# Two GpSimd drains in the expert blocks, and the second routing's constants made in the setup: one core of Trainium2

## The chip, the cores and the metric

The kernel runs on one core of a Trainium2 chip. The metric is device time in microseconds (us), taken over whole executions. The engines that matter here are TensorE (PE in the profile, its weight loads PEld), VectorE (DVE), ScalarE (ACT), GpSimd (POOL) and SyncE (SP), which issues most DMAs. A name with a q (POOLq) is an engine's sequencer: waits, branches and drains are handled there.

## The reference

Attention over 4 batches, 8 heads, 768 positions and head size 64, banded with 8 global and 96 local keys; its output is read as 3072 tokens of width 512. Two mixture-of-experts layers follow, each with 8 experts of 512x1024 and 1024x512:

```python
# layer 1: only tokens with x @ w_skip > 0, each to its argmax expert
h = np.maximum(xc[mask] @ w1[e], 0.0)
y[mask] = gate_w[mask, None] * (h @ w2[e])     # out = x + y
# layer 2: greedy over all (token, expert) logits in falling order,
# each expert takes cap = N // E = 384 tokens
order = np.argsort(-flat)
for idx in order: ...                          # assigned[tok] = e
out[mask] = np.maximum(x[mask] @ w1[e], 0.0) @ w2[e]
```

## The kernel before

The program is three blocks, one after the other. At the end of a block every engine executes a drain (it holds until the engine's older work is done) and then meets the others in a barrier; the next block starts behind it.

**Attention (block opened under L344, ends at L192).** GpSimd does nothing here but make constants, 32 small instructions, each chained to the next by a semaphore. They end with lane_grid (L405). Then it reads a flag, branches and drains.

**First experts (ends at L741).** VectorE routes the tokens, then 8 blocks of 256 rows follow, one for each expert, and behind them smaller overflow blocks of 128 rows where an expert has more than 256 tokens. The inputs here have one overflow block. All row traffic is indirect DMA issued by GpSimd in a fixed order of code: gather(k) fetches the rows of block k, scatter(k) writes its outputs (x_rows in the profile), z_scatter(k) writes the second layer's gate logits (gate_logits). The end of GpSimd's code reads: gather(E), z_scatter(E - 2), scatter(E - 1), z_scatter(E - 1), then for the overflow block scatter(E) and z_scatter(E), then waits until all have landed.

**Second experts (ends at L1371).** SyncE loads the logits back (L1478). VectorE reduces them to their largest and smallest value (L1907 to L1909), then bests() picks each token's best open expert (L1779 to L1784), needs() and three tries search a threshold with counts on TensorE, and the first expert, its token list (listed) and its weights follow from it. The 8 stretches k = 0 to 7 then run: GpSimd gathers the rows of k (L1521), issues four accumulating DMAs that make the low parts of w2 (L1533, w2_low_part), gathers for k + 1, and scatters outputs (L1527) tile by tile. During stretch k the search for expert k + 1 goes on beside the products.

**The constants of the second routing.** GpSimd makes them at the start of this block, L1498 to L1513, 17 instructions in a chain on the semaphore filled. VectorE waits for all 17 before its first bests(), TensorE before its first count. Among them are onesb and firstb, of which the program already holds equal tiles (onesb1, firstb1) from the setup.

Of the kernel before, what the change touches and what calls it, by code (L numbers as in the profile page):

```python
# [20 lines left out]
BF16 = mybir.dt.bfloat16  # L21
I32 = mybir.dt.int32
U32 = mybir.dt.uint32
AX = mybir.AxisListType
# [93 lines left out]
def build(nc, qT, kT, kI, vL, vG, n_global, n_local, w_gate1, w1a, w2a, w_gate2, w1b, w2b, flips, steps, out, x_dram, x1_dram, z_dram):  # L118
    with ExitStack() as ctx:
# [28 lines left out]
        rows2 = sb("rows2", [P, E, CAP // P], I32)  # L148
        late = ExitStack()
# [42 lines left out]
        with ExitStack() as st:  # L192
# [173 lines left out]
            def _(pool):  # L366
# [38 lines left out]
                keep_link(g.iota(lane_grid[:], [[1, P], [0, NT]], base=0, channel_multiplier=0, **iota))  # L405

# [334 lines left out]
        with ExitStack() as st:  # L741
# [128 lines left out]
            def _(pool):  # L870
# [55 lines left out]
                z_scatter(E - 2, 0)  # L926
                scatter(E - 1, 1)
# [443 lines left out]
        with ExitStack() as st:  # L1371
# [20 lines left out]
            firstb = tb("firstb", [P, E], BF16)  # L1392
            best, bestm, cmp1, pen, owner, rank1, high = (tb(x, [P, NT]) for x in ("best", "bestm", "cmp1", "pen", "owner", "rank1", "high"))
# [4 lines left out]
            left, shut, need, cnt, alive, value = (tb(x, [P, E]) for x in ("left", "shut", "need", "cnt", "alive", "value"))  # L1398
# [3 lines left out]
            fullf = tb("fullf", [P, CANDS], BF16)  # L1402
            onesb, after = tb("onesb", [P, P], BF16), tb("after", [P, P], BF16)
            lane1 = tb("lane1", [P, P], BF16)
            steps_f = tb("steps_f", [P, TRIES, CANDS])
            ids, idsf = tb("ids", [P, NT, 2], BF16), tb("idsf", [P, 2, NT])
# [19 lines left out]
            z_loaded, ended, turned, spread, filled = (sem(x) for x in ("z_loaded", "ended", "turned", "spread", "filled"))  # L1426
# [14 lines left out]
            PHASES, FILLS = E - 1, 17  # L1441
# [52 lines left out]
            def _(pool):  # L1494
                g = nc.gpsimd
                link = Chain(pool, filled)
                iota = dict(allow_small_or_imprecise_dtypes=True)
                link(g.memset(onesb[:], 1.0))  # L1498
                link(g.memset(fullf[:], 0.0))
                link(g.memset(pen[:], 0.0))  # L1500
                link(g.memset(owner[:], 0.0))
                link(g.memset(left[:], float(CAP)))
                link(g.memset(shut[:], 0.0))
                link(g.tensor_copy(firstb[:], first[:]))
                link(g.tensor_copy(alive[:], first[:]))
                for r in range(TRIES):
                    link(g.tensor_scalar(steps_f[:, r, :], lane[:, 0:CANDS], float(CANDS) ** -(r + 1), None, ALU.mult))
                link(g.tensor_tensor(masked[:, 0:P // E, :].rearrange("p t e -> p (t e)"), before[:], ident[:], ALU.add))
                link(g.tensor_scalar(after[:], masked[:, 0:P // E, :].rearrange("p t e -> p (t e)"), -1.0, None, ALU.add))
                link(g.tensor_scalar(lane1[:], lane[:], 1.0, None, ALU.add))  # L1510
                link(g.iota(idsf[:, 0, :], [[P, NT]], base=0, channel_multiplier=0, **iota))
                link(g.iota(idsf[:, 1, :], [[0, NT]], base=0, channel_multiplier=1, **iota))
                link(g.tensor_copy(ids[:], idsf[:].rearrange("p c t -> p t c")))  # L1513
                assert link.n == FILLS
# [21 lines left out]
                for k in WINDOWS:  # L1536
                    if k:
                        scatter(k - 1, TT - 1)
                    for i in range(FC // 2):
                        w2_low_part(k, i)  # L1540
                    if k < E - 1:
                        gather(k + 1)
                    for t in range(TT - 1):
                        scatter(k, t)
# [15 lines left out]
            def _(pe):  # L1560
# [93 lines left out]
                pe.wait_ge(filled, FILLS)  # L1654
# [117 lines left out]
            def _(dve):  # L1772
# [4 lines left out]
                def bests():  # L1777
# [335 lines left out]
```

## Time and profile before

| | us |
|---|---|
| median of 3 timed executions | 887.18 |
| lowest, highest of them | 886.32, 887.83 |
| the profiled execution, its own time | 885.47 |
| span of the profiled execution (first to last instruction) | 883.7 |
| mean granted TensorE clock | 0.944 of full speed |
| PE busy | 760.9 (86%) |
| DVE busy | 537.1 (61%) |
| ACT busy | 457.4 (52%) |
| POOL busy | 166.0 (19%) |

The profiled execution's own time stands 1.8 us over its span, since launch and end lie outside the span, and 1.7 us under the median. Busy shares are averages over three blocks; a block's ends are read from its timeline. Drains are no busy time in the profile: they stand only in the list of one line's instructions.

### The profile page before, as it was taken

What the parts mean: (1) busy time and instruction counts of PE and PEld (TensorE: products, weight loads), DVE (VectorE), ACT (ScalarE), POOL (GpSimd) and SP (SyncE); (2) the same over time, 40 slices, a digit from 0 to 9 for tenths busy, and PEclk for the clock granted to TensorE, in tenths of its full rate; (3) what the DMA queues carried; (4) which work ended last, traced back from release to release, by engine and by line L of the source; (5) the groups of instructions that cost most, each with busy time, mean ns of one, the idle gap of its engine ahead of it and who ended that gap; (6) DMA issues with size and microseconds to landing.
All of it is one profiled execution on the core that took longest, in us unless ns stands there. A gap on an engine that the chain in (4) does not pass through costs nothing. (4 is left out here: it accounts for less than half of the span.)

```text
span 883.7 us, 15444 instructions
## 1 busy us (share of the span) xinstructions
PE 760.9 (86%) x5529; PEld 693.0 (78%) x5529; DVE 537.1 (61%) x1441; ACT 457.4 (52%) x919; POOL 166.0 (19%) x186
## 2 busy tenths in 40 slices
PE   0899999999559999999999514999998989999994
PEld 0799999999559898999999413888887878789793
DVE  3977777776566875667655157665665757574310
ACT  2789888988424553445544003535454443536350
POOL 5000000000021121212221111131414231322321
PEclk9999999999869999999999655999999999999998
DMA  8888999997465445645443006667575766769651
GB/s 180 176 199 216 255 211 277 216 274 207 148 226 194 146 147 195 217 171 175 159 166 115 5 5 226 149 208 171 187 192 182 188 191 174 195 176 295 186 108 39
DMA packets 66041, 157.93 MB, mean 179 GB/s; under 512 B 11158, under 2 KB 14614, under 8 KB 65952
## 3 DMA queue, kind: packets, MB, share of 16 engines
q1 hardware_dynamic: 54240, 121.05, 46.8%
q0 software_dynamic: 11712, 35.73, 16.7%
q8 instruction: 51, 0.84, 0.4%
q14 instruction: 38, 0.31, 0.1%
HBM read 119.11 MB, written 23.50 MB: 161 GB/s over the span
## 5 line engine op out<-in xcount | busy, mean ns | idle before, releaser
L1606 PE MATMUL r_ph<-r_xh,r_w1h 128*128 128x384 f32 x256 | 92.0, 360 | 0.0
L557 ACT ACTIVATE pr<-pr,nmx 128x232 f32<-128x232 f32 (+1 forms) x192 | 79.9, 467 | 17.2 <-DVE nmx L653 17.2
L1606 PE MATMUL r_ph<-r_xh,r_w1l 128*128 128x384 f32 x256 | 87.7, 343 | 0.0
L1606 PE MATMUL r_ph<-r_xl,r_w1h 128*128 128x384 f32 x256 | 87.4, 342 | 0.0
L992 PE MATMUL m_ph<-m_xh,m_w1h 128*128 128x256 f32 (+1 forms) x288 | 85.1, 295 | 0.8 <-DVE m_hl L1194 0.7
L1117 ACT ACTIVATE m_hh<-m_ph 128x256 fp32r<-128x256 f32 (+1 forms) x72 | 26.8, 372 | 111.2 <-PE m_ph L992 111.2
L992 PE MATMUL m_ph<-m_xl,m_w1h 128*128 128x256 f32 (+1 forms) x288 | 82.9, 288 | 0.0
L992 PE MATMUL m_ph<-m_xh,m_w1l 128*128 128x256 f32 (+1 forms) x288 | 82.8, 287 | 0.0
L430 PE MATMUL sc<-kk,qh 128*128 128x256 f32 x192 | 58.8, 328 | 23.8 <-DVE ql L631 23.8
L653 DVE CUSTOM_DVE_ANT_0 pr<-sc,bias 128x232 f32<-128x232 f32 (+1 forms) x192 | 64.9, 374 | 19.2 <-PE sc L431 18.7
L1620 PE MATMUL r_py<-r_w2h,r_hh 128*128 128x512 f32 x192 | 76.4, 398 | 0.0
L564 ACT ACTIVATE prt<-tp 128x384 f32<-128x384 f32 (+1 forms) x128 | 65.2, 535 | 20.4 <-PE tp L443 17.0
L1620 PE MATMUL r_py<-r_w2h,r_hl 128*128 128x512 f32 x192 | 74.9, 390 | 0.0
L1620 PE MATMUL r_py<-r_w2l,r_hh 128*128 128x512 f32 x192 | 74.8, 390 | 0.0
L1903 DVE SCALAR_TENSOR_TENSOR r_hl<-r_ph,r_hh 128x384 fp32r<-128x384 f32 x64 | 35.3, 556 | 61.9 <-ACT r_hh L1723 61.2
L471 PE MATMUL op<-vo,prt 128*128 128x128 f32 x384 | 69.9, 277 | 3.3 <-DMA vp<-vG 1.5
L1709 ACT ACTIVATE r_w1h<-r_w 128x1024 fp32r<-128x1024 f32 x32 | 33.6, 1059 | 65.5 <-DMA r_w<-moe_w 65.1
L474 PE MATMUL op<-vp,prt 104*128 104x128 f32 x320 | 61.8, 274 | 0.0
L1723 ACT ACTIVATE r_hh<-r_ph 128x384 fp32r<-128x384 f32 x64 | 30.9, 485 | 56.4 <-PE r_ph L1606 55.9
L471 PEld LDWEIGHTS op<-vo,prt 128*128 128x128 f32 x384 | 55.5, 191 | 5.2 <-DMA vp<-vG 2.3
L992 PEld LDWEIGHTS m_ph<-m_xh,m_w1h 128*128 128x128 f32 x288 | 56.9, 198 | 1.5 <-ACT m_hh L1117 0.9
L992 PEld LDWEIGHTS m_ph<-m_xl,m_w1h 128*128 128x128 f32 x288 | 57.0, 198 | 0.3
(272 smaller groups left out, 1977.4 us busy)
## 6 DMA issues: line engine op xcount, KB each, us to landing
m_w<-moe_w SPq DMA_DIRECT2D x36, 512.0 KB, 6.3
row_buf<-moe_w SPq DMA_DIRECT2D x9, 2048.0 KB, 8.6
r_w<-moe_w SPq DMA_DIRECT2D x32, 512.0 KB, 5.8
r_w<-moe_w SPq DMA_DIRECT2D x8, 2048.0 KB, 9.5
r_w2l<-r_w POOLq DMA_DIRECT2D x32, 512.0 KB, 5.5
k_raw<-kI SPq DMA_DIRECT2D x32, 416.0 KB, 8.3
q_raw<-qT SPq DMA_DIRECT2D x32, 384.0 KB, 9.5
x_rows<-row_buf SPq DMA_DIRECT2D x8, 1536.0 KB, 8.5
```

The source lines that it names most:

```text
L430: nc.tensor.matmul(to, qh[s][:, hh, q], kk[s][:, hh, keys], start=True, stop=False)
L471: last = nc.tensor.matmul(o, w[:, t * P:(t + 1) * P], v_own(s, hh, i), start=True, stop=(i == 0))
L474: last = nc.tensor.matmul(o, w[0:CA, c * P:(c + 1) * P], v_band(s, hh, i - 1), start=False, stop=True)
L557: nc.scalar.activation(pr[n % PRS][:, t, lo:CW], pr[n % PRS][:, t, lo:CW], ACT.Exp, bias=nmx[n % PRS][:, t:t + 1], scale=-1.0).then_inc(ex ...
L564: nc.scalar.activation(prt[item % PRTS][:, 0:w], tp[item % 2][:, 0:w], ACT.Copy).then_inc(kept, 1)
L653: v.tensor_tensor_reduce(out=pr[n % PRS][:, t, lo:CW], in0=src, in1=bias0[:, h, :] if tile0 else bias[:, h, :], scale=-SCALE, scalar=3e38, ...
L992: last = nc.tensor.matmul(ph[m % 4][:, 0:W], w[:, c, m * P:(m + 1) * P], x[s][:, c, 0:W], start=(c == 0 and a == 0), stop=(c == KC - 1 and ...
L1606: last = nc.tensor.matmul(ph[m % 4][:, 0:CAP], w[:, c, m * P:(m + 1) * P], x[:, c, :], start=(c == 0 and a == 0), stop=(c == KC - 1 and a ...
L1620: last = nc.tensor.matmul(py[g % 2][:], h[:, c, t * P:(t + 1) * P], w[:, c, :], start=(c == 0 and a == 0), stop=(c == FC - 1 and a == 2))
L1709: nc.scalar.activation(w1h[:, c, :], w1[:, c, :], ACT.Copy).then_inc(w1_high, 1)
L1723: nc.scalar.activation(hh[:, m, :], ph[m % 4][:, 0:CAP], ACT.Relu).then_inc(h_high, 1)
L1903: v.scalar_tensor_tensor(out=hl[:, m, :], in0=ph[m % 4][:, 0:CAP], scalar=0.0, in1=hh[:, m, :].bitcast(F32), op0=ALU.max, op1=ALU.subtract ...
```

## The change

Three edits.

1. In the first-experts block GpSimd executes one explicit drain after z_scatter(E - 2) and before scatter(E - 1).
2. In the second-experts block GpSimd executes one explicit drain after the last stretch's four w2_low_part and before that stretch's three scatters (in the other stretches a gather stands at this place).
3. The constants of the second routing live in tiles of the whole program and are made by GpSimd at the end of the attention block's setup, behind lane_grid. onesb and firstb are the tiles that exist; after is made by one addition of lessb and ident in place of two instructions. The waits on filled go from VectorE and TensorE. The first bests() reads the logits themselves, without the mask of closed experts, since none is closed then.

The tile pen is now named pen2 throughout; nothing else changes by that.

```diff
@@ -146,6 +146,12 @@
+        fullf = sb("fullf", [P, CANDS], BF16)
+        pen2, owner = sb("pen2", [P, NT]), sb("owner", [P, NT])
+        left, shut, alive = (sb(x, [P, E]) for x in ("left", "shut", "alive"))
+        steps_f = sb("steps_f", [P, TRIES, CANDS])
+        after, lane1, onesb = sb("after", [P, P], BF16), sb("lane1", [P, P], BF16), onesb1
+        ids, idsf = sb("ids", [P, NT, 2], BF16), sb("idsf", [P, 2, NT])
@@ -403,6 +409,16 @@
                 keep_link(g.iota(tile_base[:], [[P, NT]], base=0, channel_multiplier=0, **iota))
                 keep_link(g.iota(slot_grid[:], [[1, SLOTS], [0, NT]], base=-SLOTS, channel_multiplier=0, **iota))
                 keep_link(g.iota(lane_grid[:], [[1, P], [0, NT]], base=0, channel_multiplier=0, **iota))
+                for dst, value in ((fullf, 0.0), (pen2, 0.0), (owner, 0.0), (left, float(CAP)), (shut, 0.0)):
+                    keep_link(g.memset(dst[:], value))
+                keep_link(g.tensor_copy(alive[:], first[:]))
+                for r in range(TRIES):
+                    keep_link(g.tensor_scalar(steps_f[:, r, :], lane[:, 0:CANDS], float(CANDS) ** -(r + 1), None, ALU.mult))
+                keep_link(g.tensor_tensor(after[:], lessb[:], ident[:], ALU.add))
+                keep_link(g.tensor_scalar(lane1[:], lane[:], 1.0, None, ALU.add))
+                keep_link(g.iota(idsf[:, 0, :], [[P, NT]], base=0, channel_multiplier=0, **iota))
+                keep_link(g.iota(idsf[:, 1, :], [[0, NT]], base=0, channel_multiplier=1, **iota))
+                keep_link(g.tensor_copy(ids[:], idsf[:].rearrange("p c t -> p t c")))
@@ -924,6 +940,7 @@
                 with pool.If(n > 0):
                     gather(E, 0)
                 z_scatter(E - 2, 0)
+                g.drain()
                 scatter(E - 1, 1)
                 z_scatter(E - 1, 1)
                 with pool.If(n > 0):
@@ -1389,21 +1406,16 @@
             work, hot, gt, taken = (tb(x, shape, BF16) for x in ("work", "hot", "over", "taken"))
-            firstb = tb("firstb", [P, E], BF16)
-            best, bestm, cmp1, pen, owner, rank1, high = (tb(x, [P, NT]) for x in ("best", "bestm", "cmp1", "pen", "owner", "rank1", "high"))
+            firstb = firstb1
+            best, bestm, cmp1, rank1, high = (tb(x, [P, NT]) for x in ("best", "bestm", "cmp1", "rank1", "high"))
             totals, incl, excl = (tb(x, [P, E, NT]) for x in ("tot", "incl", "excl"))
-            left, shut, need, cnt, alive, value = (tb(x, [P, E]) for x in ("left", "shut", "need", "cnt", "alive", "value"))
+            need, cnt, value = (tb(x, [P, E]) for x in ("need", "cnt", "value"))
-            fullf = tb("fullf", [P, CANDS], BF16)
-            onesb, after = tb("onesb", [P, P], BF16), tb("after", [P, P], BF16)
-            lane1 = tb("lane1", [P, P], BF16)
-            steps_f = tb("steps_f", [P, TRIES, CANDS])
-            ids, idsf = tb("ids", [P, NT, 2], BF16), tb("idsf", [P, 2, NT])
@@ -1493,25 +1505,6 @@
             @block.gpsimd
             def _(pool):
                 g = nc.gpsimd
-                link = Chain(pool, filled)
-                iota = dict(allow_small_or_imprecise_dtypes=True)
-                link(g.memset(onesb[:], 1.0))
-                link(g.memset(fullf[:], 0.0))
-                link(g.memset(pen[:], 0.0))
-                link(g.memset(owner[:], 0.0))
-                link(g.memset(left[:], float(CAP)))
-                link(g.memset(shut[:], 0.0))
-                link(g.tensor_copy(firstb[:], first[:]))
-                link(g.tensor_copy(alive[:], first[:]))
-                for r in range(TRIES):
-                    link(g.tensor_scalar(steps_f[:, r, :], lane[:, 0:CANDS], float(CANDS) ** -(r + 1), None, ALU.mult))
-                link(g.tensor_tensor(masked[:, 0:P // E, :].rearrange("p t e -> p (t e)"), before[:], ident[:], ALU.add))
-                link(g.tensor_scalar(after[:], masked[:, 0:P // E, :].rearrange("p t e -> p (t e)"), -1.0, None, ALU.add))
-                link(g.tensor_scalar(lane1[:], lane[:], 1.0, None, ALU.add))
-                link(g.iota(idsf[:, 0, :], [[P, NT]], base=0, channel_multiplier=0, **iota))
-                link(g.iota(idsf[:, 1, :], [[0, NT]], base=0, channel_multiplier=1, **iota))
-                link(g.tensor_copy(ids[:], idsf[:].rearrange("p c t -> p t c")))
-                assert link.n == FILLS
@@ -1540,6 +1533,8 @@
                         w2_low_part(k, i)
                     if k < E - 1:
                         gather(k + 1)
+                    else:
+                        g.drain()
                     for t in range(TT - 1):
                         scatter(k, t)
                 scatter(E - 1, TT - 1)
@@ -1651,7 +1646,6 @@
                 nc.tensor.transpose(pa[0:2, 0:P], ends[:], ident[:]).then_inc(turned, 1)
                 pe.wait_ge(ended, 2)
                 nc.tensor.matmul(pb[:, 0:2], ones[0:2, :], diag[:], start=True, stop=True).then_inc(spread, 1)
-                pe.wait_ge(filled, FILLS)
                 for r in range(TRIES):
                     count(0, r)
                     poll(0, r)
@@ -1774,19 +1768,21 @@
-                def bests():
-
-                    link(v.scalar_tensor_tensor(out=masked[:], in0=shut[:].unsqueeze(1).broadcast_to(shape), scalar=-SPAN_OUT,
-                                                in1=logits2[:], op0=ALU.mult, op1=ALU.add))
-                    link(v.tensor_reduce(best[:], masked[:], AX.X, ALU.max))
-                    link(v.tensor_tensor(work[:], masked[:], best[:].unsqueeze(2).broadcast_to(shape), ALU.is_equal))
+                def bests(of=None):
+
+                    if of is None:
+                        of = masked
+                        link(v.scalar_tensor_tensor(out=masked[:], in0=shut[:].unsqueeze(1).broadcast_to(shape), scalar=-SPAN_OUT,
+                                                    in1=logits2[:], op0=ALU.mult, op1=ALU.add))
+                    link(v.tensor_reduce(best[:], of[:], AX.X, ALU.max))
+                    link(v.tensor_tensor(work[:], of[:], best[:].unsqueeze(2).broadcast_to(shape), ALU.is_equal))
                     link(v.tensor_tensor(work[:], work[:], firstb[:].unsqueeze(1).broadcast_to(shape), ALU.mult))
                     link(v.tensor_reduce(bestw[:], work[:], AX.X, ALU.max))
 
                 def needs():
 
                     link(v.tensor_tensor(hot[:], work[:], bestw[:].unsqueeze(2).broadcast_to(shape), ALU.is_equal))
-                    link(v.tensor_tensor(bestm[:], best[:], pen[:], ALU.add))
+                    link(v.tensor_tensor(bestm[:], best[:], pen2[:], ALU.add))
@@ -1908,8 +1904,7 @@
                 start(v.tensor_reduce(ends[:, 1:2], logits2[:].rearrange("p t e -> p (t e)"), AX.X, ALU.min))
                 start(v.tensor_scalar(ends[:, 1:2], ends[:, 1:2], -1.0, None, ALU.mult))
                 dve.sem_inc(ended, 1)
-                dve.wait_ge(filled, FILLS)
-                bests()
+                bests(logits2)
                 dve.wait_ge(turned, 1)
```

The drains are sequencer instructions and show in no list of the order of work. The rest does. GpSimd at the start of the second-experts block, before (r_ marks a tile of this block; filled is the semaphore of the chain):

```order
L1498 MEMSET r_onesb 128x128
L1499 MEMSET r_fullf 128x32 [waits r2_filled]
L1500 MEMSET r_pen 128x24 [waits r2_filled]
L1501 MEMSET r_owner 128x24 [waits r2_filled]
L1502 MEMSET r_left 128x8 [waits r2_filled]
L1503 MEMSET r_shut 128x8 [waits r2_filled]
L1504 CAST r_firstb<-first 128x8 [waits r2_filled]
L1505 COPY r_alive<-first 128x8 [waits r2_filled]
L1507 TENSOR_SCALAR r_steps_f<-lane 128x32 [waits r2_filled] x3
L1508 TENSOR_TENSOR r_masked<-before,ident 128x128 [waits r2_filled]
L1509 TENSOR_SCALAR r_after<-r_masked 128x128 [waits r2_filled]
L1510 TENSOR_SCALAR r_lane<-lane 128x128 [waits r2_filled]
```

GpSimd at the same place, after: its first instruction of the block behind the barrier is the gather of the first rows.

```order
L757 UNCONDITIONAL_BRANCH [waits m1_z_scattered1,m1_scattered1,m1_scattered0,m1_z_scattered0]
L1505 UNCONDITIONAL_BRANCH [waits barrier_Pool_Activation_PE_DVE_SP_gather]
L1514 DMA r_xg<-x_rows,rows 128x512 [waits r2_x_turned,r2_listed]
L1514 DMA r_xg<-x_rows,rows 128x512 x2
```

GpSimd at the end of the setup, after, behind lane_grid, where before the flag banded was read at once:

```order
L413 MEMSET fullf 128x32 [waits setup_filled]
L413 MEMSET pen 128x24 [waits setup_filled]
L413 MEMSET owner 128x24 [waits setup_filled]
L413 MEMSET left 128x8 [waits setup_filled]
L413 MEMSET shut 128x8 [waits setup_filled]
L414 COPY alive<-first 128x8 [waits setup_filled]
L416 TENSOR_SCALAR steps_f<-lane 128x32 [waits setup_filled] x3
L417 TENSOR_TENSOR after<-lessb,ident 128x128 [waits setup_filled]
L418 TENSOR_SCALAR lane<-lane 128x128 [waits setup_filled]
L419 IOTA idsf 128x24 [waits setup_filled]
L420 IOTA idsf 128x24 [waits setup_filled]
L421 CAST ids<-idsf 128x48 [waits setup_filled]
```

Twelve rows with 14 instructions stand there that stood behind the barrier before.

VectorE at the start of the second-experts block, before:

```order
L1907 TENSOR_REDUCE r_ends<-logits 128x1 [waits r2_z_loaded]
L1908 TENSOR_REDUCE r_ends<-logits 128x1 [waits r2_init]
L1909 TENSOR_SCALAR r_ends<-r_ends 128x1 [waits r2_init]
L1779 SCALAR_TENSOR_TENSOR r_masked<-r_shut,logits 128x192 [waits r2_init,r2_filled]
L1781 TENSOR_REDUCE r_best<-r_masked 128x24 [waits r2_chain]
L1782 TENSOR_TENSOR r_work<-r_masked,r_best 128x192 [waits r2_chain]
L1783 TENSOR_TENSOR r_work<-r_work,r_firstb 128x192 [waits r2_chain]
L1784 TENSOR_REDUCE r_bestw<-r_work 128x24 [waits r2_chain]
L1914 TENSOR_REDUCE r_ends<-r_pa 2x1 [waits r2_turned,r2_chain]
```

VectorE at the same place, after:

```order
L1903 TENSOR_REDUCE r_ends<-logits 128x1 [waits r2_z_loaded]
L1904 TENSOR_REDUCE r_ends<-logits 128x1 [waits r2_init]
L1905 TENSOR_SCALAR r_ends<-r_ends 128x1 [waits r2_init]
L1777 TENSOR_REDUCE r_best<-logits 128x24 [waits r2_init]
L1778 TENSOR_TENSOR r_work<-logits,r_best 128x192 [waits r2_chain]
L1779 TENSOR_TENSOR r_work<-r_work,firstb 128x192 [waits r2_chain]
L1780 TENSOR_REDUCE r_bestw<-r_work 128x24 [waits r2_chain]
L1909 TENSOR_REDUCE r_ends<-r_pa 2x1 [waits r2_turned,r2_chain]
```

The wait on r2_filled and the masking instruction in front of r_best are gone; the other rows stand in the order they had.

## Rows read from the trace of the kernel before

**Rows 1.** The page's part 4, the chain that ended last, by line.

```profile
DMA r_w<-moe_w 9%; PE r_ph L1606 5%; DMA r_xg<-x_rows,rows 4%; PE r_py L1620 3%; ACT r_w2h L1714 2%; ACT r_w2l L1715 2%; POOL r_xg L1521 1%; DVE r_picks L1883 1%; PE r_pa L1565 1%; DVE r_hl L1903 1%; ACT r_hh L1723 1%; DVE r_cmpf L1802 0%; SPq L1468 0%; PE r_pb L1570 0%; DVE r_fullf L1807 0%
```

**Rows 2.** Queues at L741: x times, ns min/median/max, first to last start us.

```profile
L741 DVEq DRAIN  x1: 24/24/24, 499.6 to 499.6; - x1
...
L741 POOLq DRAIN  x1: 4227/4227/4227, 503.1 to 503.1; - x1
```

**Rows 3.** GpSimd's drain at the end of the program, L1371.

```profile
L1371 POOLq DRAIN  x1: 6594/6594/6594, 876.9 to 876.9; - x1
```

**Rows 4.** GpSimd's drain at the end of the attention block, L192.

```profile
L192 POOLq DRAIN  x1: 55/55/55, 16.6 to 16.6; - x1
```

**Rows 5.** GpSimd's DMA instructions by line: busy us, mean ns, idle before.

```profile
L1527 POOL DMA_INDIRECT out<-r_yo,r_homes x24 | 33.6, 1402 | 64.3 <-ACT r_yo L1729 61.0 <-issue 3.4
L1521 POOL DMA_INDIRECT r_xg<-x_rows,rows x24 | 31.5, 1313 | 116.5 <-issue 115.9 <-ACT r_yo L1729 0.6
L1533 POOL DMA_DIRECT2D r_w2l<-r_w x32 | 28.6, 893 | 87.2 <-ACT r_w2l L1715 87.2
L892 POOL DMA_INDIRECT m_xg<-x_rows,rows x17 | 19.8, 1163 | 16.2 <-issue 16.2
L908 POOL DMA_INDIRECT gate_logits<-m_zo,m_zrows x17 | 17.1, 1003 | 72.0 <-DVE m_zo L1185 69.6 <-issue 2.4
L899 POOL DMA_INDIRECT x_rows<-row_buf,rows x17 | 16.7, 983 | 122.8 <-DVE row_buf L1212 112.5 <-issue 10.2
```

**Rows 6.** Timeline of GpSimd, 461 to 513 us: start, duration in us, [idle before].

```profile
461.09 0.99 POOL L908 DMA_INDIRECT gate_logits<-m_zo,m_zrows  x1 [0.30 <-issue]
470.98 0.98 POOL L899 DMA_INDIRECT x_rows<-row_buf,rows  x1 [8.90 <-DVE row_buf L1212]
...
500.35 0.98 POOL L908 DMA_INDIRECT gate_logits<-m_zo,m_zrows  x1 [2.15 <-DVE m_zo L1185]
507.62 0.20 POOL L1498 MEMSET r_onesb<- 128x128 bf16 x1 [6.29 <-POOLq L741]
...
512.62 0.23 POOL L1513 CAST r_ids<-r_idsf 128x48 bf16<-128x48 f32 x1
```

**Rows 7.** Timeline of VectorE at the start of the second routing.

```profile
510.29 0.15 DVE L1909 TENSOR_SCALAR r_ends<-r_ends 128x1 f32<-128x1 f32 x1
512.88 0.36 DVE L1779 SCALAR_TENSOR_TENSOR r_masked<-r_shut,logits 128x192 f32<-128x192 f32 x1 [2.44 <-POOL r_ids L1513]
513.28 0.35 DVE L1781 TENSOR_REDUCE r_best<-r_masked 128x24 f32<-128x192 f32 x1
```

**Rows 8.** Timeline of TensorE at the same place.

```profile
510.55 0.37 PE L1651 MATMUL r_pa<-ident,r_ends 128*2 128x128 f32 x1 [11.26 <-DVEq L1910]
```

**Rows 9.** Timeline of VectorE in the setup.

```profile
6.15 1.43 DVE L96 TENSOR_SCALAR isg<-kpos,lims 128x360 f32<-128x360 f32 x1
7.61 0.35 DVE L97 TENSOR_SCALAR tmp<-rel 128x360 f32<-128x360 f32 x1
...
21.07 0.60 DVE L637 SCALAR_TENSOR_TENSOR bias<-dist,pen 128x128 f32<-128x128 f32 x2 [9.38 <-issue]
```

**Rows 10.** Timeline of GpSimd in the setup: a fill beside L96, and its last instruction.

```profile
6.00 1.37 POOL L387 MEMSET ql<- 64x1536 f32 x1
...
12.17 3.32 POOL L405 IOTA lane_grid<- 128x3072 bf16 x1
```

**Rows 11.** Timeline of GpSimd over the last second-expert stretch.

```profile
851.81 0.85 POOL L1533 DMA_DIRECT2D r_w2l<-r_w  x1 [1.60 <-ACT r_w2l L1715]
862.77 1.06 POOL L1527 DMA_INDIRECT out<-r_yo,r_homes  x1 [10.12 <-ACT r_yo L1729]
...
873.62 0.98 POOL L1527 DMA_INDIRECT out<-r_yo,r_homes  x1 [4.37 <-ACT r_yo L1729]
```

**Rows 12.** The page's part 6: an issue, KB, us to landing.

```profile
r_w2l<-r_w POOLq DMA_DIRECT2D x32, 512.0 KB, 5.5
```

More of the change, by code:

```diff
@@ L1424, in build @@
             polls, ranks_p = pb[:, 0:CANDS], pb[:, 128:128 + NT]
-            z_loaded, ended, turned, spread, filled = (sem(x) for x in ("z_loaded", "ended", "turned", "spread", "filled"))
+            z_loaded, ended, turned, spread = (sem(x) for x in ("z_loaded", "ended", "turned", "spread"))
             tried, met, judged, polled = (sem(x) for x in ("tried", "met", "judged", "polled"))
@@ L1439, in build @@
                 sem(x) for x in ("h_done", "h_high", "h_low", "y_done", "y_kept", "scattered"))
-            PHASES, FILLS = E - 1, 17
+            PHASES = E - 1
             POSED, ROUND_LINKS = 2 * ROUNDS + 2, 5
@@ L1823, in take @@
                     v.tensor_tensor(taken[:], hot[:], cmpb[:].unsqueeze(2).broadcast_to(shape), ALU.mult).then_inc(chosen, 1)
-                    link(v.scalar_tensor_tensor(out=pen[:], in0=cmpb[:], scalar=-SPAN_OUT, in1=pen[:], op0=ALU.mult, op1=ALU.min))
+                    link(v.scalar_tensor_tensor(out=pen2[:], in0=cmpb[:], scalar=-SPAN_OUT, in1=pen2[:], op0=ALU.mult, op1=ALU.min))
                     own()
@@ L1848, in take_rest @@
                 def take_rest():
-                    link(v.tensor_scalar(cmpb[:], pen[:], -1.0, None, ALU.is_ge))
+                    link(v.tensor_scalar(cmpb[:], pen2[:], -1.0, None, ALU.is_ge))
                     own()
@@ L2037, in general @@
                     glink = Chain(dve, gchain)
-                    glink(v.memset(pen[:], 0.0))
+                    glink(v.memset(pen2[:], 0.0))
                     glink(v.memset(owner[:], 0.0))
```

## The prediction

> **What bounds the kernel now.** I read first the page's chain that ended last [rows 1]. No engine holds it: weight loads, gathers, TensorE, ScalarE and VectorE share it in small parts, since each second-expert stretch waits for its rows and weights. So it has no one line to make faster, and the question becomes where all engines stand still together. Those places are the ends of the blocks. The reader is to look at the queues there. At the end of the first-expert block VectorE drains in 24 ns at 499.6 us, and GpSimd drains for 4227 ns from 503.1 [rows 2]. In GpSimd's timeline the last z_scatter is issued at 500.35 and the first instruction of the next block runs at 507.62, held for 6.29 us by L741 [rows 6]. At the end of the program it is the same: GpSimd drains for 6594 ns from 876.9 [rows 3], and the span ends 0.2 us behind that. Both drains lie wholly on the path. The third place is the start of the second routing: VectorE has its extremes at 510.44 (510.29 + 0.15) and waits until 512.88 for GpSimd's last constant [rows 6, 7].
>
> **What a GpSimd drain costs.** Three are seen. At L192, where GpSimd had issued no DMA, it took 55 ns [rows 4]. In the first-expert block it had issued 17 gathers, 17 scatters and 17 z_scatters, 51 DMAs; in the second-expert block 24 gathers, 24 scatters and 32 w2 DMAs, 80 [rows 5]. By these two, (6594 - 4227) / (80 - 51) = 81.6 ns for each DMA and 65 ns fixed, and the fixed part agrees with the 55 ns at no DMA. Three readings on one line with one slope is the ground of this forecast. The size of the DMAs does not enter: the 32 direct ones of 512 KB [rows 12] cost no more than the indirect ones. The count starts anew at each drain: from the start of the program the last one would have 131 DMAs behind it and come to 10.8 us, and it took 6.6. So a drain clears what it has counted, and an earlier drain in the same block takes its share from the last.
>
> **The first explicit drain.** It stands after z_scatter(E - 2), whose second half is issued at 461.09 and done at 462.08 [rows 6]. By then 17 gathers, 14 scatters and 14 z_scatters are issued, 45 DMAs: 65 + 45 x 81.6 ns = 3.74 us, so until about 466.1. GpSimd then sat idle for 8.90 us up to 470.98, waiting for VectorE [rows 6]. Behind the drain on GpSimd's queue stands only scatter(E - 1), so 4.9 us of cover are left, and without the cover the block's end would still have the idle time of the later waits. Left for the last drain are 6 DMAs (2 + 2 + 1 + 1): 65 + 6 x 81.6 = 0.56 us in place of 4.23. Saved **3.67 us**. Nothing else is late there: VectorE is in the barrier since 499.6 [rows 2].
>
> **The constants.** The whole old list runs from 507.62 to 512.85, 5.23 us [rows 6], and VectorE's wait for it goes. The new first instruction of bests() is the one that stood at 513.28, r_best; the mask of 0.36 us in front of it goes too [rows 7]. It can now start behind 510.44 with the gap of one chained instruction, 0.04 us (513.24 to 513.28 [rows 7]), and some 0.05 for the semaphore increment between them, which I estimate at one such gap: 510.5. Saved 513.28 - 510.5, about **2.7 us**. The wait that comes next is the one for the transposed extremes; TensorE makes them at 510.55 to 510.92 [rows 8], while bests() lasts beyond 511.9 even now, so it stays covered. Everything behind r_best hangs on it in a chain (the threshold, the first expert, its list, rows and weights) and moves by the same time.
>
> In the setup at most the same 5.23 us are added behind lane_grid, which ends at 15.49 [rows 10]: until 20.7 at the latest. The list is shorter now by onesb, firstb and one step of after, so I expect about 4.2 us, an end at 19.7. GpSimd has nothing more to do in that block. VectorE's next instruction is at 21.07 [rows 9]. Cost 0, with 0.4 to 1.4 us of cover. What lies there if the cover fails is seen at 6.15: L96 took 1.43 us while a fill of GpSimd ran from 6.00 to 7.37, and L97 with as many elements took 0.35 behind it [rows 9, 10], so one VectorE instruction beside GpSimd can lose 1.1 us. The Trainium skill (SBUF — State Buffer, section on SBUF's two separate sides) says that some VectorE instructions and GpSimd's share a port pair which the first takes whole; the trace agrees with 1.43 against 0.35, and since the two don't meet at 20 us, the sum is the same by the rule and by the rows.
>
> **The second explicit drain.** It stands behind the last w2 DMA, issued at 851.81 and done at 852.66 [rows 11]. Since the barrier GpSimd has then issued 24 + 32 + 21 = 77 DMAs: 65 + 77 x 81.6 ns = 6.35 us, until 859.0. That DMA is still in flight; should the drain also wait for it, it has landed at 857.3 by the median of 5.5 [rows 12], before the count is through. If the two added up it were 863.7. The next scatter is issued at 862.77 after 10.12 us of idling, the last at 873.62 [rows 11]: the first case costs nothing, the second delays a scatter that has 11 us to the last one. At the end 3 DMAs are left: 65 + 3 x 81.6 = 0.31 us in place of 6.59. Saved **6.28 us**.
>
> **The sum.** 3.67 + 2.7 + 6.28 = 12.65 us. On the profiled execution of 885.47 that gives 872.8, with the span at 871.0. That execution lies 1.7 us under the median of 887.18, so the time of several runs should be 887.2 - 12.7 = **874.5 us**. The renamed tile and the reused tiles are the same instructions on other addresses and cost 0. The 8 stretches start 6.4 us sooner with the same waits among themselves; I count no gain or loss in them.
>
> **Rivals.**
> *An explicit drain clears nothing* (or the count starts anew at the barrier, not at the drain). No trace here shows a drain in the middle of a block, and this is the forecast's one untested step. Then the last drains stay at 4.2 and 6.6 us, the explicit ones hide in idle time, and only the constants are gained: 887.2 - 2.7 = 884.5. For it speaks only that in the rows each drain has a barrier behind it. The Trainium skill (VectorE: DVE Perf Modes, The DRAIN you can't avoid) calls the drains at a program's ends boilerplate of about 12 ns, constant on all five engines; by that nothing would be there to save but the constants, the same 884.5. The trace agrees for VectorE's 24 ns and not for GpSimd's 4227 and 6594.
>
> *The setup's cover fails.* GpSimd's added instructions run longer than in the routing, or the start of VectorE at 21.07 [rows 9], before which it waits for nothing that the profile shows, moves with them. Price 1.1 us for each VectorE instruction that meets one, 1 to 3 us in all, on the first products: 875.5 to 877.5. Against it speak the 4.2 us, which end before 21.07.
>
> *A drain amid work in flight is many times dearer than one behind it.* This ends on the other side. GpSimd is held, and behind the second drain stand the three last scatters. The last must start at 873.62 and the two before it need 2.7 us with their gaps, so the drain may last until about 870.5, which is 17.8 us, or 0.23 us for each of the 77 DMAs, 2.8 times the price in the rows. Above that each microsecond is lost at the end. The other gains are eaten at 30.5 us, 0.40 for each DMA; at 0.5 it would be 38.5 us and the kernel at 874.5 + 20.7 = 895.2. Against it: at most the last four DMAs are in flight, and each lands in 5.5 us [rows 12].
>
> **How the numbers follow.** Forecast 0.85; a drain that clears nothing 0.07; the setup's cover fails 0.05; the drain that is too dear 0.03. The range takes the forecast and the failing cover: the low end is the profiled execution's 872.8 less the 0.4 that a better gap and spread may give, 872.4; the high end is the dearest failing cover, 877.5, with 0.3 for the spread of the runs (886.32 to 887.83): 877.8. The case of 884.5 is left out with the dear drain, 1 in 10. A measurement of this kernel can tell about 0.2%, 1.8 us, from no change; even 884.5 is faster by 0.3%. So faster 0.96, same 0.02, slower 0.02, where half of the dear drain's small chance falls on prices that are just eaten up.
>
> **What would show it.** Right: the queue at the end of the first-expert block has one GpSimd drain of about 3.7 us near 462 and one of 0.56 at the end; the end of the program has 0.31, and a drain of 6.35 stands near 846 (852.7 less 6.4). The idle time before the next block's first instruction falls from 6.29 to about 2.6. r_best starts within 0.1 us of the extremes. GpSimd's setup ends by 19.7, and VectorE's L637 instruction still starts near 21.1. Wrong: last drains of 4.2 and 6.6 us; a first product of the attention later than before; a scatter in the last stretch that waits for GpSimd and not for ScalarE; or stretches that differ in length from before by more than a few tenths.

## The result, and the profile after

The changed kernel takes 873.59 us (median of 4, 872.91 to 874.86), the kernel before beside it 887.24 (4 runs, 886.32 to 887.83): ratio 0.9844, 95% interval 0.9819 to 0.9870. Two later comparisons gave 0.9851 (0.9834 to 0.9869) and 0.9861 (0.9827 to 0.9895). The forecast was 874.5 us, a ratio of 0.9857. The times given are medians; the ratios with their intervals are the comparison to go by, and the quotient of two medians differs from its ratio by up to 0.2%, inside the interval.

Part 1 of the page of the changed kernel, one line of it. The profiled execution is the slowest of the four (874.86 us). Its span is 873.0 us, and PE is as busy as before in us:

```profile
PE 761.6 (87%) x5529; PEld 693.1 (79%) x5529; DVE 537.3 (62%) x1440; ACT 457.6 (52%) x919; POOL 164.3 (19%) x183
```

The drains on GpSimd's queue in the trace of after, the answers for four lines: the first explicit one (L943), the end of the first-experts block (L757), the second explicit one (L1537), the end of the program (L1388). These answer to [rows 2] and [rows 3]:

```profile
L943 POOLq DRAIN  x1: 5417/5417/5417, 463.7 to 463.7; - x1
...
L757 DVEq DRAIN  x1: 24/24/24, 502.7 to 502.7; - x1
...
L757 POOLq DRAIN  x1: 543/543/543, 506.3 to 506.3; - x1
...
L1537 POOLq DRAIN  x1: 9749/9749/9749, 847.6 to 847.6; - x1
...
L1388 POOLq DRAIN  x1: 297/297/297, 872.5 to 872.5; - x1
```

The drains on the path are 543 and 297 ns where they were 4227 and 6594. The work has moved to the explicit ones, 5417 and 9749 ns long. A drain's record can begin before the instruction in front of it does: the first explicit one is recorded from 463.7, and the z_scatter in front of it starts at 464.41. So part of each explicit drain's length is the DMA instruction in front of it, and the cost is counted from that instruction's end.

GpSimd around the first explicit drain and to the block's end (start, duration, [idle before]), the answer to [rows 6]:

```profile
464.41 0.99 POOL L924 DMA_INDIRECT gate_logits<-m_zo,m_zrows  x1 [0.30 <-issue]
474.32 0.98 POOL L915 DMA_INDIRECT x_rows<-row_buf,rows  x1 [8.91 <-DVE row_buf L1229]
...
503.52 0.98 POOL L924 DMA_INDIRECT gate_logits<-m_zo,m_zrows  x1 [2.33 <-DMA x_rows<-row_buf,rows]
```

The drain is over at 469.12 (463.7 + 5.42), and the next scatter goes out at 474.32, released by VectorE as before, with the same idle time, 8.91 us against 8.90.

VectorE at the start of the second routing, the answer to [rows 7]:

```profile
509.00 0.35 DVE L1903 TENSOR_REDUCE r_ends<-logits 128x1 f32<-128x192 f32 x1 [6.33 <-DMA logits<-gate_logits]
...
509.77 0.15 DVE L1905 TENSOR_SCALAR r_ends<-r_ends 128x1 f32<-128x1 f32 x1
510.07 0.35 DVE L1777 TENSOR_REDUCE r_best<-logits 128x24 f32<-128x192 f32 x1
```

r_best starts 0.15 us behind the end of the extremes (509.77 + 0.15). From the first reduction to r_best it is 1.07 us now.

The setup, GpSimd and then VectorE, the answer to [rows 9] and [rows 10]:

```profile
12.21 3.32 POOL L411 IOTA lane_grid<- 128x3072 bf16 x1
15.59 0.13 POOL L413 MEMSET fullf<- 128x32 bf16 x1
...
19.43 0.23 POOL L421 CAST ids<-idsf 128x48 bf16<-128x48 f32 x1
```

```profile
21.17 0.60 DVE L653 SCALAR_TENSOR_TENSOR bias<-dist,pen 128x128 f32<-128x128 f32 x2 [9.45 <-issue]
```

The list runs from 15.59 to 19.66 and VectorE starts at 21.17, 0.10 us from where it did.

GpSimd over the last stretch, the answer to [rows 11]:

```profile
847.61 0.85 POOL L1526 DMA_DIRECT2D r_w2l<-r_w  x1 [1.60 <-ACT r_w2l L1709]
858.59 1.06 POOL L1520 DMA_INDIRECT out<-r_yo,r_homes  x1 [10.12 <-ACT r_yo L1723]
864.03 1.04 POOL L1520 DMA_INDIRECT out<-r_yo,r_homes  x1 [4.39 <-ACT r_yo L1723]
869.42 0.98 POOL L1520 DMA_INDIRECT out<-r_yo,r_homes  x1 [4.35 <-ACT r_yo L1723]
```

The idle times in front of the three scatters are what they were (10.12, then 4.39 and 4.35), each released by ScalarE. Nothing waits for the drain.

**Where the time went**, by blocks of the two profiled executions, each block from barrier to barrier:

| block | before, us | after, us | difference | forecast |
|---|---|---|---|---|
| attention | 234.8 | 237.8 | +3.0 | 0 |
| first experts | 272.7 | 269.2 | -3.5 | -3.67 |
| second experts, to the end | 376.2 | 366.0 | -10.2 | -8.98 |
| span | 883.7 | 873.0 | -10.7 | -12.65 |

Two differences ask for experiments: the 3.0 us in the attention block, where the forecast was 0, and the second explicit drain, whose 8.9 us behind its DMA instruction (857.35 less 848.46) are 2.5 more than the count gives. The length of this drain is not chance: the five other kernels with the same drain here show 9728 to 9763 ns, this one 9749.

### The profile page after: what moved, and what is told of

The parts are those of the page before. It is cut to its first block and busy times, and to the rows that moved or that the text cites. A ratio compares the mean times of both kernels' runs of the same rounds, so it can differ in the third digit from the quotient of the medians.

```text
span 873.0 us, 15440 instructions
## 1 busy us (share of the span) xinstructions
PE 761.6 (87%) x5529; PEld 693.1 (79%) x5529; DVE 537.3 (62%) x1440; ACT 457.6 (52%) x919; POOL 164.3 (19%) x183
```

## The experiments

The theory is the prediction's: a GpSimd drain costs 65 ns and 81.6 ns for each DMA that GpSimd has issued since its last drain, whoever asks for it. Rivals: an explicit drain clears nothing; the setup list is not free; a drain amid work in flight is dearer. The kernels that are compared by a ratio ran on one chip.

**The drains alone.** The kernel before, with two lines added.

```diff
                 z_scatter(E - 2, 0)
+                g.drain()
                 scatter(E - 1, 1)
...
                     if k < E - 1:
                         gather(k + 1)
+                    else:
+                        g.drain()
```

> The kernel before with the two explicit drains and nothing of the constants. Count theory (a GpSimd drain costs 65 ns and 81.6 ns for each DMA since the last drain, and an earlier drain clears its share): 3.67 + 6.28 = 9.95 us faster than before, ratio 0.9888; last drains of 0.55 and 0.30 us. Rival, the gain came from the constants and from chance: the last drains may be short but the time falls by less than 5 us. For the attention block, whose end stood at 234.8 us in the trace of before and at 237.8 in that of after: if the setup list is to blame, it ends near 234.8 here; if it is chance, anywhere between.

Measured: 877.36 us against 887.84, ratio 0.9901 (0.9868 to 0.9934), 8.8 us faster (5.9 to 11.7) where 9.95 were expected; the two medians are 10.5 us apart. The drains on its queue, explicit, then at the two ends:

```profile
L927 POOLq DRAIN  x1: 5761/5761/5761, 460.6 to 460.6; - x1
...
L741 POOLq DRAIN  x1: 543/543/543, 503.3 to 503.3; - x1
...
L1372 POOLq DRAIN  x1: 296/296/296, 872.6 to 872.6; - x1
```

This settles the one untested step of the forecast: an explicit drain in the middle of a block does clear the count, and 3.68 and 6.30 us leave the path, at the places worked out.

**The constants alone.** The changed kernel with both g.drain() lines taken out.

```diff
                 z_scatter(E - 2, 0)
-                g.drain()
...
-                    else:
-                        g.drain()
```

> The changed kernel without its two explicit drains: the constants of the second routing are made in the setup, last drains stay at 4.2 and 6.6 us. Count theory: 2.7 us faster than before, ratio 0.997, and r_best starts within 0.2 us of the end of the extremes. Rival, the longer setup or the moved tiles slow the attention block by the 3.0 us seen in the trace of after: then no gain, ratio 1.000, and the attention block ends near 237.8 us again.

Measured: 884.75 us against 887.84, ratio 0.9974 (0.9956 to 0.9991), so 2.3 us faster (0.8 to 3.9) where 2.7 were expected. Its attention block ended at 236.2 us, and the drains at the ends are long again:

```profile
L757 POOLq DRAIN  x1: 4227/4227/4227, 507.1 to 507.1; - x1
...
L1387 POOLq DRAIN  x1: 6592/6592/6592, 880.0 to 880.0; - x1
```

The two parts together, 8.8 + 2.3 = 11.1 us by their ratios, agree with the 12.3 to 13.8 us of the whole change within their intervals. They don't need each other.

**DMAs in flight, or a dearer count.** The changed kernel, last stretch:

```diff
                     else:
+                        for i in range(FC // 2):
+                            pool.wait_ge(w2_low[i], 16 * E)
                         g.drain()
+                        g.drain()
```

> The changed kernel, in which GpSimd waits in the last stretch until all four w2 DMAs have landed and then executes two drains, one behind the other. In the trace of after the single drain there ended 8.9 us after its last DMA was issued, where 77 DMAs at the counted price are 6.35. If DMAs in flight make it dearer, the first of the two is now 6.35 us (6.2 to 6.5) and the second 0.06, since it has nothing to count. If instead the price for each DMA is higher in a busy block, the first one is 8.5 to 9 us here too. If a drain doesn't clear its count, the second costs as much as the first.

Measured once (872.45 us): the last w2 DMA was issued at 845.20,

```profile
845.20 0.85 POOL L1526 DMA_DIRECT2D r_w2l<-r_w  x1 [1.60 <-ACT r_w2l L1712]
```

and the two drains behind the wait:

```profile
L1539 POOLq DRAIN  x1: 6338/6338/6338, 851.9 to 851.9; - x1
...
L1540 POOLq DRAIN  x1: 46/46/46, 858.2 to 858.2; - x1
```

The first takes 6338 ns for 77 DMAs, 6.35 by the count; the second, with nothing to count, 46 ns. So the price for each DMA is the same in a busy stretch, and a drain empties the count entirely. The 2.5 us more in the changed kernel belong to the DMAs in flight. The wait was over at 851.9, 6.7 us behind the issue; carried over to the changed kernel (issue at 847.61), its last DMA lands near 854.3 and the drain is over at 857.35, 3 us later, where 6.35 would be left if the count began only then and almost nothing if it had been through. The stretches of the changed kernel's own trace agree that the data had landed by then: busy time of each engine, granted clock, busy share of the DMA engines, GB/s.

```profile
853.00:854.00 1.00, 1.00 (x6) 0.82 (x5) 0.00 (x0) 0.00 (x0) 0.00 (x0) 1.00 0.07 16
854.00:855.00 1.00, 1.00 (x6) 0.84 (x5) 0.00 (x0) 0.00 (x0) 0.00 (x0) 1.00 0.00 0
```

What a drain does in which order is not shown. The same kernel shows what a drain that ends late costs: held by the two drains, its first scatter went out 14.0 us behind the last w2 DMA, 3.0 later than in the changed kernel, and the last scatter 21.81 us behind it in both, so nothing was lost.

**Number, or bytes.** The kernel before, with 16 small DMAs more in the second-expert block:

```diff
                     if k < E - 1:
                         gather(k + 1)
+                    for j in range(2):
+                        n = 2 * k + j
+                        g.dma_start(x_dram[n:n + 1, 0:P], ones[n:n + 1, :]).then_inc(tiny, 16)
                     for t in range(TT - 1):
                         scatter(k, t)
```

> The kernel before, in which GpSimd issues 16 more DMAs of 512 bytes each, two in each second-expert stretch before its scatters, into rows of a scratch array that nothing reads any more. No explicit drain. If the price goes with the number of DMAs, the last drain counts 96 and is 65 + 96 x 81.6 ns = 7.90 us in place of 6.59. If it goes with bytes or with packets of data, 8 KB more are nothing and it stays at 6.6 us. The first-expert block's drain stays at 4.2.

Measured once, the ends of the two expert blocks:

```profile
L741 POOLq DRAIN  x1: 4225/4225/4225, 504.3 to 504.3; - x1
...
L1371 POOLq DRAIN  x1: 7905/7905/7905, 887.4 to 887.4; - x1
```

7905 ns, where 7.90 us were expected for 96 DMAs: 16 DMAs of 512 bytes added 1.31 us, 82 ns each, the price that the rows of before gave with 32 DMAs of 512 KB among them. The kernel took 897.3 us, some 9 more than before, of which the drain is 1.3. The rest is in the stretches: one gather to the next was 44.55 us there (710.63 to 755.18) and 43.30 before. The wait for a load that grew most is ScalarE's for w2, 14.7 to 19.2 us in all. In the stretches named the first two scatters go out 2.2 us before and 0.1 behind SyncE's issue of that load in the kernel before, and 1.2 before and 1.2 behind it here; that this shift is the reason is likely and not shown. It is a part of the 8 us and not all of it.

**Is the setup list free?** Three kernels. The first has the list in the setup beside the old one, into tiles that nothing reads:

```diff
                 keep_link(g.iota(lane_grid[:], [[1, P], [0, NT]], base=0, channel_multiplier=0, **iota))
+                for dst, value in ((sfullf, 0.0), (spen2, 0.0), ...
+                    keep_link(g.memset(dst[:], value))
+                keep_link(g.tensor_copy(salive[:], first[:]))
...
```

> The kernel before with the setup list of the change added behind lane_grid, into further tiles that nothing reads; the old list of the second routing and all its waits stay, and there is no explicit drain. Theory that the setup is free: the time stays that of before, ratio 0.999 to 1.001, and the attention block ends within the 234.5 to 235.7 us of the three kernels seen so far without the setup list. Theory that the list or its tiles cost something: the block ends at 236.2 to 237.8 us, as in the three kernels that have it, and the kernel is 1 to 3 us slower than before.

The second only declares those tiles:

```diff
         rows2 = sb("rows2", [P, E, CAP // P], I32)
+        sfullf = sb("sfullf", [P, CANDS], BF16)
+        spen2, sowner = sb("spen2", [P, NT]), sb("sowner", [P, NT])
...
```

> The kernel before with the further tiles declared and never written: all later tiles lie at other addresses, no instruction is added. If a later end of the attention block comes from the places of the tiles, it ends at 236.2 us or later here and the kernel is 1 to 3 us slower than before; if it comes from the instructions or from chance, it ends at 234.5 to 235.7 us and the time is that of before (ratio 0.999 to 1.001).

The third is the change with the list at another place:

```diff
                 for k in range(E - 1):
                     gather(k + 1, (k + 1) % 2)
+                    if k == 0:
+                        constants()
```

> The changed kernel with the list of constants moved out of the attention setup into the first-experts block, behind GpSimd's gather(1), where it idled for 27 us. All else as in the change. If the setup list is free where the change put it: the same time as the changed kernel beside it, within 1 us. If the setup list costs 1 to 3 us in the attention block: faster than the changed kernel by that, with the attention block's end back at 234.5 to 235.7 us.

And the change beside them:

> The changed kernel once more, on the chip of the other three, as their measure. Forecast 12.65 us faster than before, ratio 0.9857; drains of 0.54 and 0.30 us at the ends of the blocks and of 5.4 and 9.75 us where the explicit ones stand. If the attention block's end at 237.8 us was chance, it comes earlier here.

Measured: with the kernel before at 886.06 us, list added 888.27, ratio 1.0016 (0.9994 to 1.0037); tiles alone 886.60, 1.0004 (0.9992 to 1.0017); list in the first-experts block 874.36, 0.9855 (0.9834 to 0.9876); the change itself 873.50, 0.9851 (0.9834 to 0.9869). No two that differ in the list's place can be told apart. The ends of the attention block in all traces:

| | ends of the attention block, us |
|---|---|
| setup list present (7 kernels) | 237.8, 236.2, 236.3, 236.3, 236.5, 236.2, 237.1 |
| setup list absent (6 kernels) | 234.8, 234.5, 235.7, 236.5, 235.4, 235.7 |

The medians are 236.3 and 235.55, and the two lists overlap. But one thing is sharp. GpSimd's two barrier events at the end of the attention block, in the kernel before, in the one with the tiles alone, in the one with the list in the first-experts block, in the one with the list added, and in the change (first and last start):

```profile
L192 POOLq EVENT_SEMAPHORE  x2: 17/17/17, 234.7 to 234.8; - x2
```

```profile
L198 POOLq EVENT_SEMAPHORE  x2: 17/17/17, 236.4 to 236.5; - x2
```

```profile
L198 POOLq EVENT_SEMAPHORE  x2: 17/17/17, 235.3 to 235.4; - x2
```

```profile
L198 POOLq EVENT_SEMAPHORE  x2: 17/17/17, 235.8 to 236.3; - x2
```

```profile
L198 POOLq EVENT_SEMAPHORE  x2: 17/17/17, 236.0 to 236.5; - x2
```

They are 0.1 us apart in all six kernels without the list there and 0.5 in all seven with it, and every other engine waits for the second. So the list costs 0.4 us, at the barrier, some 215 us after it has run. It isn't VectorE's work, which starts at 20.9 to 21.2 us in all of these. Why GpSimd comes late to the second event is open. That it executes 14 more instructions in this block is the only difference of its code between the kernel with the list added and the one with the tiles alone. The traces do show the queues that carry instructions, and one packet of them (queue q14) moves with the list: it goes at 240 to 242 us in all seven kernels with it and at 250 to 253 in all six without. Neither instruction queue (q8, q14) moves anything from 3 us before the block's end to 1.5 behind it, so no transfer seen there explains the 0.4 us. Of the other 2.6 of the 3.0 us between the two first profiles, 0.6 stand in TensorE's drain at the block's end: 1815 ns in the change, 1713 in the kernel with the tiles alone, and 1205 to 1208 in the eleven others, so this part is not the list's. The remaining 2.0 are left open. Kernels whose attention code is the same end it up to 2.0 us apart (234.5 to 236.5), so chance can be most of it; the timed comparison of the added list, from 0.5 us faster to 3.3 slower, can't say more.

**A drain where nothing covers it.** The changed kernel, all stretches:

```diff
                     if k < E - 1:
                         gather(k + 1)
-                    else:
-                        g.drain()
+                    g.drain()
```

> The changed kernel with a drain at that place of every second-expert stretch, behind the gathers of the next one, not of the last alone. Each now counts about 10 DMAs, 0.88 us by the counted price. In stretches 0 to 6 three gathers are in flight, which land 3.4 to 4.5 us after their issue; in stretch 7 the last w2 DMA is, which lands some 6 us after it. If a drain goes through its count and waits for what is in flight, those of stretches 0 to 6 last 4 to 6 us and the one of stretch 7 ends when its DMA lands, about 6 us after its start and not 9.75. The scatters behind them go out 3 to 5 us later, into the load of w2: 1 to 2 us for each of 7 stretches, 7 to 14 us slower than the changed kernel. If a drain doesn't wait for DMAs in flight, each lasts 2 us with the last gather's issue and the time stays that of the changed kernel within 2 us.

Measured: 883.42 us against 886.95, ratio 0.9963 (0.9948 to 0.9978), where the change had 0.9861 beside it: 9 us slower than the change. It was slower by what was expected if a drain waits. Its eight explicit drains, then the one of stretch 0 and the one of stretch 7 by themselves:

```profile
L1536 POOLq DRAIN  x8: 6138/6289/7504, 574.8 to 855.7; - x8
...
L1536 POOLq DRAIN  x1: 6152/6152/6152, 574.8 to 574.8; - x1
...
L1536 POOLq DRAIN  x1: 6877/6877/6877, 855.7 to 855.7; - x1
```

GpSimd in stretch 0, the last gather and the scatter, and in stretch 7 the last w2 DMA:

```profile
576.67 1.55 POOL L1514 DMA_INDIRECT r_xg<-x_rows,rows  x1 [0.30 <-issue]
581.90 1.02 POOL L1520 DMA_INDIRECT out<-r_yo,r_homes  x1 [3.68 <-issue]
...
855.76 0.85 POOL L1526 DMA_DIRECT2D r_w2l<-r_w  x1 [1.60 <-ACT r_w2l L1708]
```

In stretch 0 the drain's record begins at 574.8, before the second and the third gather instruction do (575.32 and 576.67). The last of them is done at 578.22, and the scatter goes out 3.68 us behind it, where 0.30 us lay between them before. The count of about 10 DMAs gives 0.88 us of that; the rest is a wait for what is in flight: the drain that began at 574.8 and took some 6.2 us was over at 581, 4.3 us behind the start of the last gather, and gathers landed 3.4 to 4.5 us behind their start in the trace of before. In stretch 7 the drain, with 7 DMAs to count (0.64 us), lasted 6.9 us from the issue of the last w2 DMA, about the 6.7 that such a DMA took to land in the kernel with the wait. So behind a landing almost nothing is left of a count of 7, and 3 us are left of a count of 77. The row of waits for w2, of the change and of this kernel (total, times, longest):

```profile
ACT r_w2h L1708 <- DMA r_w<-moe_w: 14.9, 7, 2.6
```

```profile
ACT r_w2h L1707 <- DMA r_w<-moe_w: 20.1, 7, 3.4
```

The later scatters meet the load of w2, and this wait is 5 us longer than in the change; for the other 4 of the 9 us no row is shown. All of the 9 lie in the stretches: from the first gather to the last scatter they took 344.9 us here and 334.7 to 335.5 in the three traces of the change.

**More of the same.** Two more drains, and the list in the first-experts block:

```diff
                 z_scatter(E - 1, 1)
+                g.drain()
...
+                g.drain()
                 scatter(E - 1, TT - 1)
```

> The changed kernel with three things more: the constants made in the first-experts block behind gather(1), a drain behind z_scatter(E - 1), and a drain in front of the very last scatter. Behind them 2 DMAs and 1 DMA are left for the drains at the ends of the blocks: 65 + 163 = 0.23 us in place of 0.54, and 0.15 in place of 0.30. With the 0.4 us between GpSimd's two barrier events at the end of the attention block, which only kernels with the longer setup show, 0.9 us faster than the changed kernel, if the last scatter isn't held: its drain counts 2 DMAs and has 4.35 us of idle time, but waits for a scatter in flight that lands up to 4 us after its issue. If that costs more than its cover, the last scatter starts later than the 1.5 us behind ScalarE's copy that it needs now, and the gain is gone.

> The changed kernel beside the other two, as their measure: ratio to the kernel before 0.985.

Measured: 874.77 us and 0.9863 (0.9833 to 0.9893), the change beside it 875.63 and 0.9861 (0.9827 to 0.9895). The queue, added drain and end of each block:

```profile
L951 POOLq DRAIN  x1: 3247/3247/3247, 486.0 to 486.0; - x1
...
L746 POOLq DRAIN  x1: 212/212/212, 504.2 to 504.2; - x1
...
L1546 POOLq DRAIN  x1: 3922/3922/3922, 860.3 to 860.3; - x1
...
L1394 POOLq DRAIN  x1: 128/128/128, 869.1 to 869.1; - x1
```

The drains on the path fell to 212 and 128 ns, and the barrier events of the attention block are 0.1 us apart. That is 0.33 + 0.17 + 0.4 = 0.9 us off the path by the profile; the timed runs can't show it. Before the last scatter the added drain took 3.92 us, in a gap of 4.38 that ScalarE still ended.

## Why the prediction was right

**The price of a drain** was right in its size and in its kind. Two rows gave 81.6 ns; 6 DMAs came to 543 ns (0.56 expected), 3 to 297 (0.31), 96 to 7905 (7.90), 77 landed ones to 6338 (6.35), 2 and 1 to 212 and 128 (0.23, 0.15). That size doesn't enter follows from the rows of before too: with 55 ns for no DMA, the 51 indirect ones come to 81.8 ns each, and what is then left for the 32 of 512 KB to 81.6. The cumulated count was excluded from rows of before alone, and so it proved. One reading in a rival was loose: VectorE's 24 ns were taken to agree with a drain of constant length, but its three drains in the trace of before are 24, 42 and 301 ns, and TensorE's 72, 1123 and 1208. At the ends of the two expert blocks GpSimd's is the last to be over.

**The first explicit drain**: from the end of the DMA instruction in front of it (465.40) to 469.12 it took 3.72 us, 3.74 expected. Saved 3.68, 3.67 expected. The prediction's end at 466.1 was a slip: 462.08 + 3.74 is 465.8, so 5.2 us of cover and not 4.9, and 5.2 were left (469.12 to 474.32). Here two z_scatters were in flight, which land 2.1 us behind their issue in the trace of before (the middle value), and they added nothing to the count.

**The constants**: from the first reduction to r_best 3.77 us before and 1.07 after, 2.70 saved, 2.7 expected. The gap was 0.15 and not 0.09 us, which the rounding took up.

**The setup**: the list ended at 19.66 (19.7 expected) and VectorE was not touched. The cost of 0 was wrong by the 0.4 us at the barrier. The prediction looked for a price where the list runs, beside VectorE, and had none for the place where it showed.

**The second explicit drain** is the term that was mis-sized: 6.35 us expected and 8.9 measured behind its DMA instruction. The failing step is "it has landed before the count is through", taken to mean that the two overlap wholly. The other case, both added up, was named as a bound and gave 863.7 in the time of before, which is 11.0 us; the truth lay between. It cost nothing, since the cover was 10.12 us, but 1.2 us of cover were left and not 3.8.

**The rival of a drain that is dear amid work in flight** has its mechanism, in small: it waits for landings, 3 us behind the last gather where the count gives 0.9. In the place chosen it took 8.9 us, far below the 17.8 from which it would have decided (18.3 by the prediction's own terms, since 873.62 less 2.7 is 870.9 and not 870.5). The same drain in every stretch costs 9 us, since there the queue behind it isn't idle.

**The sum**: 12.65 us forecast, 12.3 to 13.8 by the three ratios. Term by term, the profiles give 3.68 + 2.70 + 6.30 less 0.4, 12.3 us. The intervals of the three ratios reach 1.6 to 3.0 us to either side, so that the forecast met the median within 1 us is partly luck. In the profiled execution the second-expert block was 1.2 us shorter than its terms say. Of this 0.8 lie between the first gather and the last scatter, 335.5 us before and 334.7 after. The eleven kernels other than those with sixteen more DMAs and with a drain in every stretch took 332.5 to 337.6 us there, so 0.8 is no more than chance; the sign of a wrong forecast that asked for "a few tenths" asked for more than one execution can tell.

## What to carry to other kernels

Read the drains at the ends of blocks on GpSimd's own queue: they stand in no busy share, and each DMA that GpSimd has issued adds to them. Where GpSimd idles later than most of its DMAs and before the last ones, an explicit drain moves that cost off the path. Give it enough cover, which is the time for which GpSimd's queue idles behind it anyway: the count's time plus the landing of what is in flight is the safe sum, and none of the drains worked out here took more. Look at what stands behind it on the queue: in a gap it is free, in front of work that others wait for it costs more than it saves.

## What the runs showed of the hardware

A drain with nothing to clear takes 46 to 58 ns, and one DMA adds 82 ns whether it moves 512 bytes or 512 KB. A drain waits for DMAs in flight, and this adds to the count in part: 2.5 us for 77 DMAs with the last one 6.7 us from landing, and nothing for 45 with the last one some 2.1 us from it. Fourteen more small instructions of GpSimd in a block, long over, put 0.4 us more between its two events at that block's barrier, in seven kernels of seven; why is open.
